# Searching for a capacity bound in three rounds of 63, 127 and 127 candidates instead of four rounds of 31

## The reference

```python
# 1. a linear attention with a decaying state, batch 4, 8 heads, 768 steps, width 48
x = attention(r, k, v, w, u)                 # -> 3072 tokens of 384
# 2. a mixture of 8 experts: every token goes to the expert of its largest logit
h = relu(x[mask] @ w1[e]); out[mask] = gate * (h @ w2[e])
# 3. a second mixture of 8 experts, each with room for exactly 384 tokens
logits = x @ w_gate                          # 3072 x 8
for idx in argsort(-logits.flatten()):       # best pair of token and expert first
    tok, e = idx // 8, idx % 8
    if assigned[tok] >= 0 or counts[e] >= 384: continue
    assigned[tok] = e; counts[e] += 1
h = relu(x[assigned == e] @ w1[e]); out[assigned == e] = h @ w2[e]
```

## Time and profile before

| | |
|---|---|
| median of three runs | 867.92 us (866.15 to 871.0) |
| the profiled execution | 872.95 us |
| its span | 871.2 us |
| TensorE busy (PE) | 825.2 us, 95% of the span |
| TensorE's weight loads (PEld, beside the matmuls) | 605.4 us, 69% |
| VectorE (DVE) | 432.5 us, 50% |
| ScalarE (ACT) | 319.3 us, 37% |
| GpSimd (POOL) | 123.8 us, 14% |
| granted TensorE clock, mean | 0.968 of full speed |

### The profile page before, as it was taken

How to read it: one execution, slowest core, us unless ns; L and a number is a source line. 1 busy time by engine, 2 the same in 40 slices (tenths; PEclk the granted TensorE clock), 3 DMA queues, 4 the chain that set the end, 5 groups by cost and what they waited for, 6 DMA issues and landing times. The chain is left out here.

```text
span 871.2 us, 18195 instructions
## 1 busy us (share of the span) xinstructions
PE 825.2 (95%) x6388; PEld 605.4 (69%) x6389; DVE 432.5 (50%) x1257; ACT 319.3 (37%) x808; POOL 123.8 (14%) x148
## 2 busy tenths in 40 slices
PE   8999999959999999999999983999999999999996
PEld 7888888757887778887778862755555565565653
DVE  8899999642333333333333337663636365453000
ACT  4878787714334444334443330111111212122120
POOL 5123433320000000000000000103111020211201
PEclk9999999969999999999999995899999999999998
DMA  9455555636557565557474420532415052345100
GB/s 317 147 176 184 187 178 186 251 124 241 176 210 245 172 216 180 185 214 245 171 241 142 160 100 1 173 104 96 164 38 181 19 182 78 131 154 199 38 19 29
DMA packets 61920, 136.23 MB, mean 156 GB/s; under 512 B 4696, under 2 KB 36320, under 8 KB 61856
## 3 DMA queue, kind: packets, MB, share of 16 engines
q1 hardware_dynamic: 45824, 98.87, 32.8%
q0 software_dynamic: 6912, 23.75, 8.0%
q10 hardware_dynamic: 9120, 12.77, 4.7%
HBM read 117.48 MB, written 17.89 MB: 155 GB/s over the span
## 5 line engine op out<-in xcount | busy, mean ns | idle before, releaser
L1370 PE MATMUL p_o<-w2s,hid_t 128*128 (+1 forms) x432 | 156.8, 497 | 0.0
L1354 PEld LDWEIGHTS p_h<-x_t,w1s 128*128 128x128 f32 x1296 | 150.9, 192 | 7.8 <-issue 1.1
L1354 PE MATMUL p_h<-x_t,w1s 128*128 128x128 f32 x1296 | 153.4, 275 | 0.7 <-issue 0.7
L1828 PE MATMUL p_go<-w2s,g_hid 128*128 128x384 f32 x384 | 136.9, 500 | 0.0
L1812 PE MATMUL p_gh<-g_t,w1s 128*128 128x384 f32 x384 | 135.1, 496 | 0.0
L1370 PEld LDWEIGHTS p_o<-w2s,hid_t 128*128 128x128 f32 x432 | 75.8, 190 | 41.2 <-issue 5.2
L1207 ACT ACTIVATE hid_t<-p_h 128x512 f32<-128x512 f32 x54 | 32.2, 597 | 187.0 <-PE p_h L1354 181.2
L1828 PEld LDWEIGHTS p_go<-w2s,g_hid 128*128 128x128 f32 x384 | 70.8, 193 | 41.0 <-issue 1.7
L1812 PEld LDWEIGHTS p_gh<-g_t,w1s 128*128 128x128 f32 x384 | 69.7, 190 | 42.0 <-issue 2.7
L1570 ACT ACTIVATE g_hid<-p_gh 128x384 f32<-128x384 f32 x64 | 31.4, 490 | 120.6 <-PE p_gh L1812 120.6
L1530 POOL DMA_INDIRECT g_in<-y_rows,table x24 | 24.0, 1002 | 257.5 <-DVE table L1685 252.7
(11 more groups left out here) (267 smaller groups left out, 1162.4 us busy)
## 6 DMA issues: line engine op xcount, KB each, us to landing
w1s<-in_w SPq DMA_DIRECT2D x28, 1536.0 KB, 6.6
kr_t<-in_kr_t SPq DMA_DIRECT2D x24, 512.0 KB, 3.9
w1s<-in_w1b SPq DMA_DIRECT2D x8, 1536.0 KB, 6.7
w2s<-in_w2b SPq DMA_DIRECT2D x8, 1536.0 KB, 10.3
w2s<-in_w POOLq DMA_DIRECT2D x12, 768.0 KB, 6.9
w_pad<-in_w_t SPq DMA_DIRECT2D x24, 256.0 KB
v_pad<-in_v_pad SPq DMA_DIRECT2D x24, 256.0 KB, 4.2
x_in<-sorted_rows ACTq DMA_DIRECT2D x28, 198.0 KB, 2.5
```

The source lines that it names most:

```text
L1354: ins = pe.matmul(p_h[g][:, m, :], w1s[:, q, a, f:f + P], x_t[:, q, a, :], start=(a == 0), stop=(a == KD - 1))
L1370: ins = pe.matmul(p_o[:, :], hid_t[:, m, :], w2s[:, bass.ds(half, 1), m, :].rearrange("p o n -> p (o n)"), start=(m == 0), stop=(m == KF - 1))
L1828: ins = pe.matmul(p_o[n % 2][:, :], hid[:, m, i * P:(i + 1) * P], w2s[:, p % 2, m, :], start=(m == 0), stop=(m == KF - 1))
```

## The change

From the third phase on (p = 2 to 6) the search has three rounds, of 6, 7 and 7 bits, which is 20 bits as before; the first two phases keep four rounds of 5 bits. `cand`, `cand_n` and `reach` are large enough for 127 candidates, the semaphore targets count the rounds through `ASKED`, and the steps of VectorE and TensorE take their sizes from `cands(p, k)`. A second set of shares is made in phase 1, in four small VectorE instructions. `read_table` stands ahead of `find_takers` in phase 2 too. TensorE's order is written anew from phase 2 on, with one pattern for all phases.

```diff
-QUICK = 4
-CAND = 2 ** 5 - 1
 PHASES = E - 1
+CLOSE = 2
+FAR, NEAR = (5, 5, 5, 5), (6, 7, 7)
+DIGITS_OF = [FAR if p < CLOSE else NEAR for p in range(PHASES)]
+ASKED = [sum(len(digits) for digits in DIGITS_OF[:p]) for p in range(PHASES)]
+
+def cands(p, k):
+    return 2 ** DIGITS_OF[p][k] - 1
...
-    cand = sb("cand", [P, CAND], F32)
-    reach = sb("reach", [P, SLOTS, CAND], BF16)
+    cand = sb("cand", [P, 2 ** 7 - 1], F32)
+    reach_all = sb("reach", [P, SLOTS * (2 ** 7 - 1)], BF16)
+    reach = lambda n: reach_all[:, 0:SLOTS * n].rearrange("p (s c) -> p s c", c=n)
...
             def offer(p, k):
-                size, start = sizes[:, k:k + 1], (low if k else floor)[:, 0:1]
+                n, size, start = cands(p, k), sizes[:, k:k + 1], (low if k else floor)[:, 0:1]
                 if p + k > 0:
-                    step(dve.tensor_scalar(cand[:, :], cand_n[:, :], size, start, ALU.mult, ALU.add))
-                dve.tensor_tensor(reach[:, :, :], wide(free(p)[:, :], CAND),
-                                  cand[:, :].unsqueeze(1).broadcast_to([P, SLOTS, CAND]), ALU.is_ge).then_inc(s_reach, 1)
+                    step(dve.tensor_scalar(cand[:, 0:n], cand_n[:, 0:n], size, start, ALU.mult, ALU.add))
+                dve.tensor_tensor(reach(n), wide(free(p)[:, :], n),
+                                  cand[:, 0:n].unsqueeze(1).broadcast_to([P, SLOTS, n]), ALU.is_ge).then_inc(s_reach, 1)
...
+                if p == 1:
+                    for k in range(len(NEAR)):
+                        step(dve.memset(near_shares[:, k:k + 1], 2.0 ** -sum(NEAR[0:k + 1])))
+                    step(dve.tensor_scalar(near_of_floor[:, :], near_shares[:, :], floor[:, 0:1], None, ALU.mult))
                 narrow(p, 2)
-                offer(p, 3)
-                narrow(p, 3)
+                if p < CLOSE:
+                    offer(p, 3)
+                    narrow(p, 3)
...
-                    if p == 0:
+                    if p in (0, 2):
                         read_table(p)
                         find_takers(p + 1)
...
             def count(p, k):
-                pe.wait_ge(s_reach, QUICK * p + k + 1)
+                n = cands(p, k)
+                pe.wait_ge(s_reach, ASKED[p] + k + 1)
                 for i in range(SLOTS):
-                    ins = pe.matmul(p_c[0:CAND, :], reach[:, i, :], takers[:, i, :], start=(i == 0),
+                    ins = pe.matmul(p_c[0:n, :], reach(n)[:, i, :], takers[:, i, :], start=(i == 0),
                                     stop=(i == SLOTS - 1))
...
             tables(1)
-            second(0, range(10, 18))
+            second(0, range(10, 19))
             count(2, 0)
-            second(0, range(18, 19))
-            digit(2, 0)
             second(0, range(19, 20))
             for i in range(TE):
                 x_transposes(1, i)
+                if i == 1:
+                    digit(2, 0)
                 second(0, range(20 + i, 21 + i))
             second(0, range(23, 24))
...
+            for p in range(2, PHASES):
+                second(p - 1, range(7, 17))
+                if p < PHASES - 1:
+                    count(p + 1, 0)
+                for i in range(TE):
+                    second(p - 1, range(17 + 2 * i, 19 + 2 * i))
+                    if i == 0 and p < PHASES - 1:
+                        digit(p + 1, 0)
+                    x_transposes(p, i)
+                second(p - 1, range(23, 24))
+                if p == PHASES - 1:
+                    break
+                first(p, range(0, 4))
+                count(p + 1, 1)
+                first(p, range(4, 6))
+                digit(p + 1, 1)
+                first(p, range(6, 14))
                 count(p + 1, 2)
+                first(p, range(14, 16))
                 digit(p + 1, 2)
+                first(p, range(16, 18))
                 total(p + 1)
+                first(p, range(18, 22))
                 rank(p + 1)
+                first(p, range(22, 24))
+                second(p, range(0, 7))
                 tables(p + 1)
```

More of the change, by code:

```diff
@@ L366, in _ @@
             const(pool.iota(keep["tokid"][:, :], pattern=[[0, 1]], base=0, channel_multiplier=1, **small))
[L367 removed]
+            const(pool.iota(keep["cand_n"][:, :], pattern=[[1, 2 ** 7 - 1]], base=1, channel_multiplier=0, **small))
             const(pool.iota(keep["iota_p"][:, :], pattern=[[1, P]], base=0, channel_multiplier=0, **small))
@@ L1625, in narrow @@
-                dve.wait_ge(s_digit, QUICK * p + k + 1)
+                n, size, start = cands(p, k), sizes[:, k:k + 1], (low if k else floor)[:, 0:1]
+                dve.wait_ge(s_count, ASKED[p] + k + 1)
+                step(dve.tensor_tensor(filled[0:n, :], p_c[0:n, :], (room if p else room0)[0:n, :], ALU.is_ge))
+                dve.tensor_reduce(hit[0:n, :], filled[0:n, :], AX.X, ALU.max).then_inc(s_hit, 1)
+                dve.wait_ge(s_digit, ASKED[p] + k + 1)
                 step(dve.tensor_scalar(low[:, :], p_d, size, start, ALU.mult, ALU.add))
@@ L1836, in _ @@
             pe.matmul(p_m[:, 0:1], ones[0:1, :], bound[0:1, :], start=True, stop=True).then_inc(s_bound, 1)
-            for k in range(QUICK):
+            for k in range(len(FAR)):
                 count(0, k)
@@ L1877, in _ @@
                 x_transposes(1, i)
+                if i == 1:
+                    digit(2, 0)
                 second(0, range(20 + i, 21 + i))
             second(0, range(23, 24))
-            first(1, range(0, 1))
+            first(1, range(0, 4))
             count(2, 1)
-            first(1, range(1, 2))
+            first(1, range(4, 6))
             digit(2, 1)
-            first(1, range(2, 5))
+            first(1, range(6, 14))
             count(2, 2)
-            first(1, range(5, 6))
+            first(1, range(14, 16))
@@ L1887, in _ @@
             digit(2, 2)
[L1888 to L1892, removed]
+            first(1, range(16, 18))
             total(2)
-            first(1, range(13, 17))
+            first(1, range(18, 22))
             rank(2)
-            first(1, range(17, 24))
-            second(1, range(0, 3))
+            first(1, range(22, 24))
+            second(1, range(0, 7))
             tables(2)
-            second(1, range(3, 11))
@@ L1924, in _ @@
+                second(p, range(0, 7))
                 tables(p + 1)
-                first(p, range(23, 24))
-                second(p, range(0, 8))
-                if p + 2 < PHASES:
-                    count(p + 2, 0)
-                    second(p, range(8, 9))
-                    digit(p + 2, 0)
-                    second(p, range(9, 13))
-                    count(p + 2, 1)
-                    second(p, range(13, 14))
-                    digit(p + 2, 1)
-                    second(p, range(14, 17))
-                else:
-                    second(p, range(8, 17))
@@ L1938, in _ @@
-                for i in range(TE):
-                    x_transposes(p + 1, i)
-                    second(p, range(17 + 2 * i, 19 + 2 * i))
-                second(p, range(23, 24))
             p = PHASES - 1
```

35 lines of the change are left out of this document (14 added, 21 removed).

## The result

The kernel after is slower: a median of 870.81 us (869.39 to 872.0, five runs) against 866.54 for the kernel before (865.58 to 871.0, five runs), a ratio of 1.0041 with a 95% interval of 1.0023 to 1.0059. I had forecast 866.3, a gain of 1.6 on the median of 867.92 that the kernel before had after three runs; two more brought it to 866.54. The time lies inside the range, 856 to 874, and the direction is wrong. By the bounds of the prediction (slower above 872.3) the change would count as none, but the interval leaves out 1.

A forecast was written before the change was run, and what follows sets the result against it. The prediction took TensorE, busy 95% of the span, to bound the kernel. Its terms, −6.8 + 9.0 + 0.3 + 1.5 + 0.14 − 6.7 + 1.0, gave −1.6 us: 866.3 us from a median of 867.92, range 856 to 874.

The forecast's parts named there:

- (f): First digits of phases 2 and 3: TensorE's waits and clock loss vanish, −6.7 us, with +1.0 for waits that return.
- the clock's part was the profiled execution's luck: Bound for the lost stretches of phases 2 and 3: only −2.9 us regained, the two waits without the clock.
- (a): One search round less in each of phases 2 to 6, 1.36 us of TensorE each: −6.8 us.
- (b): Ten counts of 127 candidates: slow weight loads make each 1.77 us, +0.90 each, +9.0 us.
- (c): Five first rounds with 63 candidates: 30 ns a load with its moving columns, +0.06 each, +0.3 us.
- (d): `tables` nine units after `rank`: TensorE waits 0.3 us for the second half of `row_is`, five times, +1.5 us.
- (e): VectorE's longer `reach`, 4.26 us at 127 candidates: covered by TensorE's units with 0.2 us to spare, except 0.14 once.
- Phase 2's 0.14: In phase 2 seven units and one transpose, 5.14 us, cover `reach` too briefly: 0.14 us late, once.
- the fast load: Rival: weight loads of 127 columns in the counts are fast, −0.9 us there, 856.4 us in all; chance 0.20.
- the doubled one: Rival: a weight column in the counts costs twice as much, +26 us for 127 candidates, 887.6 us; chance 0.08.
- The clock did not fall behind the long counts: Denies the rival that TensorE's clock falls once a phase behind long counts, +9.5 us, 875.9 us; chance 0.10.
- The late compares: Rival: GpSimd's `put` behind the gathers delays compares in phases 3 to 6, 0.9 us each, 869.0 us; chance 0.14.

The follow-up runs named there:

- a_best: The kernel after with 128 weight columns in every count from phase 2 on and `tables` one unit later: 859.67 us, 0.9855 of before.
- experiment 5: The kernel after with `tables` one unit later, ten units behind `rank`, in phases 2 to 6: 871.28 us, 0.9989 of before.
- b_late: The kernel before with six small VectorE instructions ahead of the first compare of phases 2 and 3: 880.25 us, 1.0084 of before.
- b_128: The kernel before with its counts from phase 1 on loading 128 columns of weights instead of 31: 868.62 us, 0.9956 of before.

## Why the prediction was wrong

**The step that failed is (f).** I took "all 6.7 us as gone, −6.7", with +1.0 for what comes back, so −5.7 in all. In the usual execution, on every chip where before takes some 867 us, there was nothing to regain: five of six profiles of before have none of the two waits. The prediction even had the hint: it says that the median lies 5.0 us below the profiled execution, and carried the sum over as if both had lost the same. It priced the case too ("the clock's part was the profiled execution's luck"), but only for the clock's part and not for the waits. Without (f) its own sum is −6.8 + 9.0 + 0.3 + 1.5 + 0.14 = +4.1, and the medians moved by 4.3. That this comes so close is in part luck, since several terms were off and cancel out, as follows.

(a), the price of a round, was right where it was read; (b), +9.0 for the long loads: forecast 1.77 us a count and 139 ns a load, measured 1.79 and 139. The reading of three load lengths on one line decided it.

(c) was too small: a count of 63 takes 1.09 us, not 0.93, so +1.1 in place of +0.3. Its load, 113 ns, is near the line (79 + 0.47 x 63 = 109); 31 pairs at 35 ns instead of 30 are more than the line gives.

(a) and (b) together were too large by the slow starts. A round of 127 costs 728.36 − 719.92 − 10 x 0.645 = 1.99 us, where I had 1.36 + 0.90 = 2.26. Two units ahead of such a digit take 1.38 us (721.71 to 723.09), 0.09 more than two units alone, where one unit ahead of a digit of 31 rows takes 0.2 more. Behind a digit that reads 127 rows the next unit is free after 0.03 us (723.09 to 723.12), where it took 0.10 behind one of 31 rows. Ten times 0.27 is −2.7.

(d) had the right place. Its waits are 1.1 us in place of 1.5, but a `tables` in two parts costs more than the wait: from first row to next product the five take 1.11, 1.12, 1.12, 1.47 and 0.87 us where they took 0.78, 1.8 us more in all. (e) was right: 4.265 us for `reach`, and no wait of TensorE at the counts. Phase 2's 0.14 didn't show as a wait.

Together: undisturbed before 253.17, after 256.46, a change of +3.3 us in the stretch, against +4.1 forecast without (f). I added up TensorE's rows of both stretches by kind, each from its start to the next start and less 0.645 us for each unit. The rounds cost 27.1 us against 26.3, +0.8 where (a), (b) and (c) have +2.5. `tables` costs +1.8. The transposes and the products just behind them cost 8.5 against 7.8, +0.7, for which the prediction has no term: the new order puts a digit ahead of them, and the first transpose behind it takes 0.38 us where the others take 0.33 (712.85 to 713.24 in the profile of after); the first products of the next expert start slower too. These three are the 3.3.

Of the rivals, the fast load is refuted and so is the doubled one, both by 1.79 us. The clock did not fall behind the long counts in any profile of after: it is 1.00 from 558 to 855 us in all four. The late compares did come back in kernels with the new order (digits that wait 0.86 us twice and 0.47 in a_best, 0.45 and 0.48 in experiment 5), in several phases and with the clock untouched, as that rival said, but only on the holding chip.

## What to carry to other kernels

Hold the profiled execution's own time against the timed runs before pricing anything in it: a loss as large as the difference between the two may be absent from the median, and a second profile shows it. Where the kernel before takes other times on another chip, compare on both. When a bf16 weight tile has nearly 128 columns, load exactly 128, even if the rest is neighbours' data whose sums nobody reads: here one column decided between a loss of 0.4% and a gain of 0.8%. Fewer and longer search rounds pay off only where the engine that carries the path doesn't pay for their length.

## What the runs showed of the hardware

- A bf16 weight load takes 94 ns for 31 columns, 113 for 63, 139 for 127 and 96 for 128; 31 such loads with 8 moving columns take 0.87, 1.09, 1.79 and 0.78 us.
- GpSimd's indirect DMAs that start while a long VectorE instruction with two inputs in SBUF is running are stretched: those beside `reach` in the kernel after end 0.8 to 0.9 us after it. One that starts ahead of it is not (588.97, 0.95 us, `reach` from 589.34). A scatter of 1 us took 4.86:

```profile
597.06 4.26 DVE L1630 TENSOR_TENSOR reach<-free_best,cand 128x3937 bf16<-128x3937 f32 x1
...
597.33 4.86 POOL L1552 DMA_INDIRECT out<-o_row,table  x1 [2.41 <-DMA out<-o_row,table]
```

  It ends 0.87 us after `reach`. The Trainium skill, "SBUF — State Buffer", section "SBUF: two separate sides", has an exclusive lock on a port pair that the two engines share, which a VectorE instruction with two SBUF inputs holds against a GpSimd instruction that reads SBUF. This row agrees, if an indirect DMA counts as one, which no run here tells. It cost nothing in this profile, since nobody waited for the scatter.
- The other direction depends on the chip or the execution. On the holding chip all four profiles had VectorE instructions that started 0.3 to 2.1 us after the count they waited for, each 0.3 to 1.1 us behind the end of one of GpSimd's indirect DMAs. On three other chips none was over 0.11 us late, with the same instructions at the same distances. The kernel before took 873.8 us on the one and 867.2 to 867.7 on the others. The chip alone may not be all: the first profile of the kernel before had late compares too, beside timed runs of 865.58 to 871.0, and which chip it ran on is not on record. What makes the difference stays open.
- TensorE's granted clock fell to 0.50 behind waits of 1.35 and 1.52 us (first profile) and of 3.1 us (b_late), and stayed at 1.00 behind waits of 1.49 and 1.70 (b_128).
